# Moving the tails' projections of eleven head pairs next to the queries' in a kernel of linear attention and two expert layers

## The reference

```python
# 4 batches, 8 heads, 576 tokens, head dimension 64, 128 features
scale = 64 ** -0.25
def phi(x):                                  # x: [b, h, s, 64]
    h = einsum('bhsd,md->bhsm', x, omega) - sum(x * x) / 2
    return exp(h - max(h)) / sqrt(128)
q_p, k_p = phi(q * scale), phi(k * scale)
kv, z = einsum('bhsm,bhsd->bhmd', k_p, v), sum(k_p, axis=2)
attn = (q_p @ kv) / (q_p @ z + 1e-6)         # [b, h, s, 64]
x = attn as [2304 tokens, 512]
h = x @ w_in;   x = (h * clip(h + 3, 0, 6) / 6) @ w_out      # w_in 512x2048
h = x @ w_in2;  out = (h * sigmoid(1.702 * h)) @ w_out2
```

## Time and profile before

| what | value |
|---|---|
| median of 3 runs | 944.45 us (943.81 to 944.54) |
| profiled execution, its time | 943.76 us |
| its span, first to last instruction | 941.3 us |
| TensorE (PE) busy | 932.8 us, 99% |
| TensorE weight loads (PEld) busy | 782.8 us, 83% |
| DVE busy | 394.3 us, 42% |
| ACT busy | 380.5 us, 40% |
| POOL busy | 169.9 us, 18% |
| granted TensorE clock, mean | 1.000 of full speed |

### The profile page before, as it was taken

How to read it: one execution, slowest core, us unless ns; L and a number is a source line. 1 busy time by engine, 2 the same in 40 slices (tenths; PEclk the granted TensorE clock), 3 DMA queues, 4 the chain that set the end, 5 groups by cost and what they waited for, 6 DMA issues and landing times.

```text
span 941.3 us, 12974 instructions
## 1 busy us (share of the span) xinstructions
PE 932.8 (99%) x5126; PEld 782.8 (83%) x5126; DVE 394.3 (42%) x735; ACT 380.5 (40%) x871; POOL 169.9 (18%) x182
## 2 busy tenths in 40 slices
PE   8999999999999999999999999999999999999998
PEld 7878878887888778888889988888888888888898
DVE  6755565555546554452233432232223222422322
ACT  7765655545445444432225642232223222322322
POOL 3656554212221210000006820000000000000000
PEclk9999999999999999999999999999999999999999
DMA  8534341211122110010003600000001000100000
GB/s 276 179 92 145 95 142 27 63 50 52 26 63 64 38 51 13 1 46 1 1 0 107 179 30 1 1 12 34 0 1 46 1 1 0 45 1 1 10 36 24
DMA packets 40731, 45.99 MB, mean 49 GB/s; under 512 B 21600, under 2 KB 22240, under 8 KB 40672
## 3 DMA queue, kind: packets, MB, share of 16 engines
q1 hardware_dynamic: 40304, 44.54, 15.7%
q10 hardware_dynamic: 368, 0.62, 0.2%
HBM read 40.44 MB, written 4.72 MB: 48 GB/s over the span
## 4 chain that ended last, share of the span: by engine, by line
PE 96%; DVE 2%; ACT 2%; issue 0%; DVEq 0%
PE acc L616 14%; PE acc L617 14%; PE acc L618 14%; PE hid L593 11%; PE hid L597 10%; PE hid L594 10%; PE att L593 4%; PE att L594 4%; PE att L597 4%; PE att L519 3%; PE att L482 3%; PE att L561 2%; PE att L504 1%; PE att L475 1%; DVE row_max L864 1%; PE acc L482 0%
## 5 line engine op out<-in xcount | busy, mean ns | idle before, releaser
L616 PE MATMUL acc<-g_hi,w_out_hi 128*128 128x512 f32 (+1 forms) x640 | 241.5, 377 | 0.1
L618 PE MATMUL acc<-g_hi,w_out_lo 128*128 128x512 f32 (+1 forms) x640 | 236.2, 369 | 0.0
L617 PE MATMUL acc<-g_lo,w_out_hi 128*128 128x512 f32 (+1 forms) x640 | 236.0, 369 | 0.0
L593 PE MATMUL hid<-x_hi,w_in_hi 128*128 128x512 f32 (+1 forms) x476 | 181.6, 381 | 0.0
L597 PE MATMUL hid<-x_lo,w_in_hi 128*128 128x512 f32 (+1 forms) x476 | 176.0, 370 | 0.4 <-DVE x_lo L974 0.4
L594 PE MATMUL hid<-x_hi,w_in_lo 128*128 128x512 f32 (+1 forms) x476 | 175.4, 369 | 0.0
L989 DVE TENSOR_TENSOR g_lo<-R,g_hi 128x512 fp32r<-128x512 f32 (+1 forms) x160 | 108.0, 675 | 92.4 <-ACT g_hi L762 92.4
L616 PEld LDWEIGHTS acc<-g_hi,w_out_hi 128*128 128x128 f32 x640 | 120.7, 189 | 21.8 <-issue 2.4
L618 PEld LDWEIGHTS acc<-g_hi,w_out_lo 128*128 128x128 f32 x640 | 120.7, 189 | 20.6
L617 PEld LDWEIGHTS acc<-g_lo,w_out_hi 128*128 128x128 f32 x640 | 120.8, 189 | 19.4
L762 ACT ACTIVATE g_hi<-R 128x512 fp32r<-128x512 f32 (+1 forms) x160 | 94.6, 591 | 84.3 <-DVE R L984 52.6
(11 more groups left out here) (143 smaller groups left out, 1042.3 us busy)
## 6 DMA issues: line engine op xcount, KB each, us to landing
X<-w_in SPq DMA_DIRECT2D x16, 256.0 KB, 2.7
X<-w_out SPq DMA_DIRECT2D x16, 256.0 KB, 3.2
out_t<-X SPq DMA_DIRECT2D x16, 256.0 KB, 2.3
q_cols<-q_t SPq DMA_DIRECT2D x14, 288.0 KB, 2.9
k_cols<-k_t SPq DMA_DIRECT2D x14, 288.0 KB, 3.6
rows<-q_n SPq DMA_DIRECT2D x13, 288.0 KB, 3.5
rows<-k_n SPq DMA_DIRECT2D x13, 288.0 KB, 3.2
v_rows<-v_n SPq DMA_DIRECT2D x14, 256.0 KB, 3.3
```

Source lines behind the costliest of these rows:

```text
L593: nc.tensor.matmul(bank, w_hi[0][:, at], x_hi[:, k, x0:x0 + t], start=(k == 0), stop=False)
L616: nc.tensor.matmul(bank, w_hi[1][:, at], g_hi[:, g, 0:t], start=(s == 0), stop=False)
L617: nc.tensor.matmul(bank, w_hi[1][:, at], g_lo[:, g, 0:t], start=False, stop=False)
L618: last = nc.tensor.matmul(bank, w_lo[1][:, at], g_hi[:, g, 0:t], start=False, stop=(s == J - 1))
```

## The change

The list of units gives each slot a tuple now. The tail's projection moves from its own slot to the slot of q, directly behind q, and its old slot stays empty. The edits in the two other engines keep the tail's statistics and exponentials where they were in those engines' own orders (in the round behind the slot of q, ahead of g_lo and behind g_hi). Nothing is added or taken away, no transfer is moved in SP's or POOL's order, and pairs 0 to 4 are as before. There are 11 later pairs.

```diff
-UNITS = ("q", "tail", "k", "turn0", "turn1", "kv", "nd0", "nd1")
+UNITS = (("q", "tail"), (), ("k",), ("turn0",), ("turn1",), ("kv",), ("nd0",), ("nd1",))
...
                 if 0 <= at < SLOTS_A_PAIR:
-                    units.append((a, UNITS[at]))
+                    units += [(a, u) for u in UNITS[at]]
...
# scalar engine
                 for a, what in former:
                     if what in ("q", "k"):
                         exps(a, what, 0)
-                    else:
+                    elif what != "tail":
                         attend(a, what)
                 gate(n)
...
                     exps_of(LEAD - 1, "tail")
+                for a, what in former:
+                    if what == "tail":
+                        attend(a, what)
                 for a, what in now:
                     if what not in ("nd0", "nd1"):
...
# vector engine
                     statistics(LEAD - 1, "tail")
+                for a, what in former:
+                    if what == "tail":
+                        attend(a, what)
                 for a, what in now:
                     if what == "nd0":
```

## The result

| | before | after |
|---|---|---|
| median, 19 runs each | 944.45 us (943.45 to 945.57) | 942.41 us (941.9 to 943.23) |
| ratio, after to before | | 0.9979 (95% interval 0.9972 to 0.9986) |
| profiled execution, its time | 943.76 us | 941.9 us |
| its span | 941.3 us | 939.4 us |

The kernel became 0.21% faster, 2.0 us in the medians and 1.9 us in the spans. That is just at the bound of 0.2% that the prediction names, and the interval reaches over it on both sides.

What follows compares the result with a forecast made beforehand. Bound: the rate at which PE takes matmuls. Saving one entry and exit in 11 pairs gives 2.5 us, less 0.66 for two waits: 1.8 us, so 944.45 becomes 942.6 us (chance 0.67), full range 941.5 to 943.6.

Steps and rivals of the forecast that it cites:

- bound of 0.2%: What a measurement can tell from no change, 1.9 us; chances: faster by more 0.46, within it 0.50, slower 0.04.
- What a unit costs besides its matmuls: On PE, entry 0.08 plus exit 0.14 us per projection unit; merging q and tail saves 0.23 a pair, 2.5 in all.
- The exit behind the longer unit: Behind q and tail together on PE, the exit was taken as that behind the tail alone, 0.14 us.
- bound (a): Exit behind q and tail at most 0.27 us, as behind nd1: 0.13 more a pair, leaving 1.0 us gain.
- Rival 2: The unit's cost stays, its exit growing with length: 1.0 or 0.4 us gain left, 943.5 to 944.1; chance 0.09.
- The seam: From q to tail on PE: 1.09 us start to start, as from k to tail in pair 0; 0.09 its own.
- bound b: The seam from q to tail might be free: 0.09 us a pair, 1.0 us in all, on top.
- The two waits: At hidden(17) and hidden(33), PE waits for DVE's product, pushed back 0.58 us at chunk ends: 0.33 each, 0.66 lost.
- Rival 1: No wait at the chunk ends, the chain having unseen slack: full 2.5 us gain, 942.0 us; chance 0.20.
- Rival 3: k's projection waits in every pair for q's exponentials, pushed back with ACT's gate: slower, 947.9 us at 2.0 us; chance 0.04.
- k's wait: k's projection needs q's second bank of exponentials: about 1.0 us left, called the tightest deadline in an ordinary pair.

## Why the prediction was right

The forecast was 942.6 us, and 942.41 was measured; the span was forecast at 939.5 and came out at 939.4. The mechanism came out as forecast too, with two small errors that cancel. That the span is met to 0.1 us is in part luck: pair 5's q starts at 67.40 and 67.36 us in the two profiled executions, and in others up to 1.7 us later. The stretch, 1.86 us shorter where 1.8 was forecast, is the sound measure.

- **What a unit costs besides its matmuls.** The parts came out at 1.09, 0.58, 2.86 and 2.81 us against 1.09, 0.59, 2.86 and 2.80. The period of four rounds was forecast to fall from 30.40 to 30.17 us and is 30.18, in eight of ten periods; for pairs 8 and 12 it is 30.46, forecast 30.5. The gain in a pair is 0.22 us. The 0.23 of the sum, 7.57 less 7.34, comes of starts rounded to 0.01 us: 30.40 less 30.18 is the better figure.
- **The exit behind the longer unit** did not grow to the 0.27 us of bound (a): 2.86 us for the hidden part leaves 0.14. Rival 2 is out by the trace.
- **The seam** (bound b) costs what the earlier trace rows show, and the experiment with the other tile shape gives the reason.
- **The two waits.** They stand where the prediction put them, at hidden(17) and hidden(33), and nowhere else in the stretch. The chain moved by the 0.58 us of the sum. Rival 1 is out. The term was mis-sized a little: I had the first matmul 0.10 us behind DVE's end, from output(0), and it came 0.05 us behind (172.98 to 173.03). So a wait costs 0.28 us and not 0.33. These two small errors, 11 x 0.01 too much gain and 2 x 0.05 too much loss, cancel. That it is these waits that hold back the gain is shown: without them the stretch is 0.56 us shorter, and in the two pairs by themselves the change is worth nothing.
- **Rival 3**, the wait of k's projection for q's exponentials, did not come: 0.98 us are left in all pairs, as forecast.
- **A deadline that the prediction did not see.** It called k's wait, with 1.0 us left, the tightest in an ordinary pair. It is not: in the round behind k's slot of pair 7, which ends no chunk, two slow biases on DVE leave 0.40 us between the product and hidden(13) in the kernel before (138.37 to 143.28, shown above), less than the 0.58 at hidden(17). That no third wait came is luck as far as the sum goes. The chain there starts again with k's projection, so that only the saving of 0.22 us counts against it, and 0.20 us were left (product to 142.38, hidden(13) at 142.58).
- **The sign against the bound of 0.2%.** I gave 0.46 to faster by more than that and 0.50 to no more. The ratio of 0.9979 lies at the bound, and its interval reaches from 0.14% to 0.28%. This case does not tell which was the better guess.

## What to carry to other kernels

In a stream of matmuls without gaps, the cost of a small piece of work put between them is its own length plus an entry and an exit. Read both from distances of starts: the parts around it against the same part where nothing stands between. Merging two pieces saves one entry and one exit at most, and how much of it is left differs with what is merged (0.22 us here for two projections, 0.05 for two sets of transposes).

Moving work ahead on the bound engine delays what that engine would have done in between. Add that delay and the saving itself, 0.58 + 0.23 here, and hold the sum against every deadline of the chain behind it. Look first in the rounds that carry extra work: the two at chunk ends had 0.48 us before the move. But look at every round: of the nine ordinary pairs eight had some 1.0 us or more left after the move, and one, with two slow instructions on DVE, had 0.20 us.

When the chain is late, look for an early step that stands behind a late one for no reason of data. The gate waited only because of its place in ACT's order.

## What the runs showed of the hardware that I had not expected

- How the exit's 0.14 us is spread. In the changed kernel the hidden part behind q and tail takes 2.86 us against the 2.72 of the earlier trace rows. The distance from its first matmul to its second is 0.34 us, 0.11 more than further on, and the remaining 0.03 us spreads over the next few. I have no experiment on the reason.
- A bias on 128x2 elements took 1.21 us on DVE in the run with the tail in front of k, while POOL had its subtraction on 128x512 elements running (137.62 to 138.91). The same operation takes 0.17 us at 167.95 in the changed kernel. It is no single case. In the traces of the ten executions here, 128 of the 960 instructions that make `h_max` and `bias` took over 0.25 us. Each of these had a POOL instruction in flight and ended 0.01 to 0.03 us behind the end of one. Of the 690 that had none in flight, none was slow; 142 with one in flight were not slow either. That DVE is held up until POOL is done fits all of them, but no run here takes POOL's work away.
- The start of the later pairs varies by 1.8 us between executions of kernels that are equal up to there: 67.3 to 69.1 us. It is decided in the first 12 us, by pair 0. There q's 16 instructions took 1.16 to 1.18 us in the kernels that reached pair 5 at 67.3 to 67.4 (the changed kernel, 1.33 and 67.36, nearly so), 1.38 in the one at 67.68, and 1.83 to 2.08 in those at 68.0 us or later. In the latest, the tail in front of k with the gate first, k's 16 took 2.08 us too. First the kernel before, then that one:

```profile
4.49 1.18 PE L482 MATMUL acc<-omega,q_cols 64*128 64x128 f32 x16
6.15 1.16 PE L482 MATMUL acc<-omega,k_cols 64*128 64x128 f32 x16 [0.48 <-DMA k_cols<-k_t]
```

```profile
4.44 2.08 PE L482 MATMUL acc<-omega,q_cols 64*128 64x128 f32 x16
7.48 2.08 PE L482 MATMUL acc<-omega,k_cols 64*128 64x128 f32 x16 [0.96 <-DMA k_cols<-k_t]
```

The wait for k's columns is not what decides it, as it is 0.75 and 0.93 us in two of the kernels that started early (67.36 and 67.33). Why the same instructions take nearly twice as long there is open: the granted clock is 1.00 of full speed in these stretches in all the traces. For differences of 0.5 us a stretch read from the trace was a far better measure here than the span or a median of some ten runs.
